# Attention and two gated layers on one core: score products by half tiles, one half ahead, and inverses handled by pairs of tiles

## What is computed

```
scores = scale * q @ k.T + bias          # bias: -slope[head] * distance, masked to -1e9
a = exp(scores - max); a = a / (sum(a) + 1e-9)
x = (a @ v), heads joined                          # [2, 768, 512]
gate = sigmoid(causal conv over 5 positions of x)
x = (gate * (x @ w_val)) @ w_out
h = relu(x @ w_in)
gate = sigmoid(conv over 3 positions of h)
out = (h * gate) @ w_out2
```

## Time and profile before

| | us |
|---|---|
| median of 3 runs | 261.65 (261.6 to 261.84) |
| the profiled execution, device time | 260.86 |
| its span, first to last instruction | 259.1 |
| first turned tile on PE | 35.92 |
| `pv(10)` starts on PE | 87.02 |
| `val_part(0, 0)` starts on PE | 89.14 |
| PE busy in the whole span | 248.1 (96%) |

### The profile page before, as it was taken

The page is one execution under the profiler, slowest core; times in us unless marked ns, Lnnn a source line. Parts: engine busy times, 40 slices in busy tenths (PEclk is TensorE's granted clock), DMA queues, the critical chain, the costliest instruction groups (busy, mean ns, idle before and its releaser), DMA issues.

```text
span 259.1 us, 4771 instructions
## 1 busy us (share of the span) xinstructions
PE 248.1 (96%) x1702; PEld 199.7 (77%) x1702; DVE 183.4 (71%) x469; ACT 147.8 (57%) x346; POOL 46.8 (18%) x71
## 2 busy tenths in 40 slices
PE   8999989989789899999999999999999999999995
PEld 7644558888688778888888888888888888888883
DVE  0388369998989988989805969986139989990000
ACT  1061649999999854455517058855458559662100
POOL 1002255777478612000000000000000000000000
PEclk9999999999999999999999999999999999999999
DMA  6799957897976120000000000000000004004021
GB/s 204 266 341 270 287 199 202 248 239 229 271 220 202 57 74 4 0 4 0 0 0 3 0 0 0 1 3 0 0 0 3 0 0 162 3 0 162 0 115 47
DMA packets 24636, 24.69 MB, mean 95 GB/s; under 512 B 3732, under 2 KB 16532, under 8 KB 24484
## 3 DMA queue, kind: packets, MB, share of 16 engines
q1 hardware_dynamic: 23460, 23.37, 29.8%
q10 hardware_dynamic: 1152, 1.01, 1.2%
HBM read 21.03 MB, written 3.34 MB: 94 GB/s over the span
## 4 chain that ended last, share of the span: by engine, by line
PE 84%; ACT 9%; DVE 5%; issue 2%
PE ps L592 21%; PE ps L594 21%; PE ps L593 21%; PE ps L478 9%; ACT prob L732 6%; PE ps L559 3%; DVE prob L982 3%; PE ps L525 2%; PE ps L563 2%; ACT probT L739 2%; PE ps L493 2%; PE ps L489 1%; DVE probT L989 1%; DVE xT L1005 1%; ACT Wh L720 0%
## 5 line engine op out<-in xcount | busy, mean ns | idle before, releaser
L732 ACT ACTIVATE prob<-prob,low 128x232 f32<-128x232 f32 (+1 forms) x96 | 44.2, 465 | 4.9 <-DVE low L982 4.8
L1010 DVE SCALAR_TENSOR_TENSOR g<-xT,cw,g 128x512 f32<-128x512 f32 x48 | 34.7, 787 | 1.6 <-ACT g L767 1.6
L838 ACT ACTIVATE h<-ps 128x512 f32<-128x512 f32 x24 | 14.0, 596 | 31.2 <-PE ps L594 31.1
L982 DVE CUSTOM_DVE_ANT_0 prob<-ps,bias 128x232 f32<-128x232 f32 x80 | 28.0, 388 | 1.5 <-PE ps L525 1.5
L559 PE MATMUL ps<-probT,v_new 128*64 128x128 f32 x192 | 19.3, 280 | 6.5 <-ACT probT L739 6.5
L592 PE MATMUL ps<-gh,Wh 128*128 128x512 f32 x64 | 24.9, 389 | 0.0
L593 PE MATMUL ps<-gl,Wh 128*128 128x512 f32 x64 | 24.9, 389 | 0.0
L594 PE MATMUL ps<-gh,Wl 128*128 128x512 f32 x64 | 24.9, 389 | 0.0
L592 PE MATMUL ps<-hghA,w2h 128*128 128x512 f32 x64 | 24.9, 389 | 0.0
L593 PE MATMUL ps<-hglA,w2h 128*128 128x512 f32 x64 | 24.9, 389 | 0.0
L594 PE MATMUL ps<-hghA,w2l 128*128 128x512 f32 x64 | 24.9, 389 | 0.0
(11 more groups left out here) (110 smaller groups left out, 590.1 us busy)
## 6 DMA issues: line engine op xcount, KB each, us to landing
q_rows<-in_q SPq DMA_DIRECT2D x12, 256.0 KB, 4.3
kW<-in_k SPq DMA_DIRECT2D x12, 256.0 KB, 5.4
v_new<-in_v SPq DMA_DIRECT2D x12, 240.0 KB
invT<-inv_turned SPq DMA_DIRECT2D x20, 128.0 KB, 3.4
out<-xT SPq DMA_DIRECT2D x5, 512.0 KB, 2.8
w<-in_w SPq DMA_DIRECT2D x8, 256.0 KB, 9.3
v_old<-in_v SPq DMA_DIRECT2D x10, 192.0 KB
prob<-in_wval SPq DMA_DIRECT2D x1, 1024.0 KB, 4.9
```

The source lines that it names most:

```text
L732: act.activation(part, part, ACT.Exp, scale=-1.0, bias=low[:, t % 2, i:i + 1], accum_out=total[:, t % 2, i, 0:1]).then_inc(exp_done, 1)
L838: act.activation(h_cols(m, c), pieces(HB(m), c), ACT.Relu).then_inc(relu_done, 1)
L982: dve.tensor_tensor_reduce(prob[:, t % 2, i, cols], SC(f, e)[:, i % HH // 2, cols], table, -SCALE, 3.0e38, ALU.add, ALU.min, low[:, t % 2, ...
L1010: dve.scalar_tensor_tensor(out=pieces(g[:, m, :], c), in0=x_cols(m, c, tap - PAD1), scalar=cw1[:, m, tap:tap + 1], in1=pieces(g[:, m, :], ...
```

## The change

Scores are made by half tiles. PE no longer starts an iteration with the scores of tile t+1. It turns tile t, makes the first half of the scores of tile t+2, does `pv(t)`, and then makes the second half of tile t+2. DVE reads the four heads of the first half of tile t+2 at the end of iteration t, ahead of `take_x(t)`, so its iterations begin with the copies of the turned tile. The inverses of two tiles are made, stored and spread together, in odd iterations on DVE and SP; POOL scales two tiles in even iterations, starting at 2. `total` has four slots in place of two. ACT's order is not changed.

```diff
             def send_inverses(u):
+                slot = u % 2
+                sp.wait_ge(inverse_done, u + 1)
+                sp.dma_start(inv_turned[u].rearrange("h (b q) -> b h q", q=SQUARE), inv_rows[:, slot, :]).then_inc(inv_sent[slot], 16)
+
+            def spread_inverses(u):
+                slot = u % 2
+                sp.wait_ge(inv_sent[slot], 16 * (u // 2 + 1))
+                if u >= 1:
+                    sp.wait_ge(x_ready, 2 * u)
                 for e in range(2):
-                    sp.dma_start(invT_of(t)[e * D:(e + 1) * D, :, :], inv_turned[t, e:H:2, :].partition_broadcast(D)).then_inc(invT_in[slot], 16)
+                    sp.dma_start(invT_of_two(u)[e * D:(e + 1) * D, :, :], inv_turned[u, e:2 * H:2, :].partition_broadcast(D)).then_inc(invT_in[slot], 16)
...
                 for t in range(TILES):
-                    send_inverse(t)
+                    if t % 2 == 1:
+                        send_inverses(t // 2)
                     if t >= 1 and t - 1 + RING < TILES:
                         load_v(t - 1 + RING)
                     if t + RING < TILES:
                         load_q(t + RING)
                         load_k(t + RING)
-                    spread_inverse(t)
+                    if t % 2 == 1:
+                        spread_inverses(t // 2)
...
-                    if t >= 1:
+                    if t >= 2 and t % 2 == 0:
+                        scale_x(t - 2)
                         scale_x(t - 1)
+                scale_x(TILES - 2)
                 scale_x(TILES - 1)
...
                 for t in range(TILES - 1):
-                    if t >= 1:
-                        qk(t + 1)
                     for f in range(HALVES):
                         turn(t, f)
+                    if t + 2 < TILES:
+                        qk_half(t + 2, 0)
                     pv(t)
+                    if t + 2 < TILES:
+                        qk_half(t + 2, 1)
...
+                for i in range(HH):
+                    score(1, i)
                 for t in range(TILES - 1):
-                    if t >= 1:
-                        take_x(t - 1)
-                    score(t + 1, 0)
-                    score(t + 1, 1)
-                    inverse(t)
-                    score(t + 1, 2)
-                    turn_inverse(t)
                     copy_t1(t, 1)
-                    score(t + 1, 3)
+                    if t % 2 == 1:
+                        inverses(t // 2)
                     copy_t1(t, 3)
+                    if t % 2 == 1:
+                        turn_inverses(t // 2)
                     for i in range(HH, H):
                         score(t + 1, i)
+                    if t + 2 < TILES:
+                        for i in range(HH):
+                            score(t + 2, i)
+                    take_x(t)
                     for _ in range(EARLY_STEPS.get(t, 0)):
                         early_conv1(next_step)
                         next_step += 1
-                take_x(TILES - 2)
-                inverse(TILES - 1)
-                turn_inverse(TILES - 1)
+                inverses(TILES // 2 - 1)
+                turn_inverses(TILES // 2 - 1)
```

More of the change, by code:

```diff
@@ L125, in program @@
         low = sb("low", [P, 2, H], where=am)
-        total = sb("total", [P, 2, H, 2], where=am)
-        total_eps = sb("total_eps", [P, H], where=am)
+        total = sb("total", [P, 4, H, 2], where=am)
+        total_eps = sb("total_eps", [P, 2, H], where=am)
         inv = sb("inv", [P, SQUARE], where=am)
@@ L135, in program @@
         attention_memory.close()
[L136 removed]
+        inv_turned = nc.dram_tensor("inv_turned", (TILES // 2, SQUARE, P), f32, kind="Internal").ap()
         gm = ExitStack()
@@ L511, in _, with qk_half @@
             product_W(CT + 1)
+            def qk_half(t, f):
+                slot = t % RING
+                if f == 0:
+                    pe.wait_ge(q_in[slot], landed(t))
+                    pe.wait_ge(k_in[slot], landed(t))
+                    pe.wait_ge(k_window, k_windows(t))
+                if t >= 1:
+                    pe.wait_ge(score_done, H * (t - 1) + HH * (f + 1))
+                for i in range(HH):
+                    pair, rows = 2 * f + i // 2, slice(i % 2 * D, i % 2 * D + D)
+                    keys = kW[rows, slot, pair, OLD if first_of_batch(t) else 0:KEYS]
+                    last = pe.matmul(SC(f, i % 2)[:, i // 2, OLD if first_of_batch(t) else 0:KEYS], q_rows[rows, slot, pair, :], keys,
+                                     start=True, stop=True)
+                last.then_inc(qk_done, 1)
             def qk(t):
-                slot = t % RING
-                pe.wait_ge(q_in[slot], landed(t))
-                pe.wait_ge(k_in[slot], landed(t))
-                pe.wait_ge(k_window, k_windows(t))
                 for f in range(HALVES):
-                    if t >= 1:
-                        pe.wait_ge(score_done, H * (t - 1) + HH * (f + 1))
-                    for i in range(HH):
-                        pair, rows = 2 * f + i // 2, slice(i % 2 * D, i % 2 * D + D)
-                        keys = kW[rows, slot, pair, OLD if first_of_batch(t) else 0:KEYS]
-                        last = pe.matmul(SC(f, i % 2)[:, i // 2, OLD if first_of_batch(t) else 0:KEYS], q_rows[rows, slot, pair, :], keys,
-                                         start=True, stop=True)
-                    last.then_inc(qk_done, 1)
+                    qk_half(t, f)
             def turn_bank(t, j):
```

41 lines of the change are left out of this document (17 added, 24 removed).

## The result

The changed kernel takes **264.94 us** (median of 4 runs, 263.04 to 267.02), the kernel before, on the same chip in the same minutes, 261.62 (4 runs, 260.95 to 261.84). The ratio is 1.0119, with a 95% interval of 1.0081 to 1.0157. So the change costs some 1%, where I had forecast a gain of 0.5%. A second measurement, made later with six runs, gave 262.87 against 260.77, a ratio of 1.0092 (1.0056 to 1.0127): again slower, by somewhat less. All ratios here leave out executions more than 1.5% above the fastest of their kernel (here the one of 267.02 us), so they are not quite the quotients of the medians.

What follows compares the result with a forecast made beforehand. ACT, nearly full, bounds the attention loop. 2.5 us won, less 0.2 (late DVE copies), 0.3 (convolution beside POOL) and 0.8 (key windows), gives 1.2: 261.65 - 1.2 = 260.4 us, range 259.2 to 262.0.

Steps and rivals of the forecast that it cites:

- What bounds the loop, and what can be won: Attention loop: ACT nearly full, 4.67 us of work in rounds of 5.03; at most 2.5 us to win.
- Window 6: POOL's key window for tile 6: done at 56.8, wanted at 54.8, PE stands 2.0, 0.8 us lost.
- Later ones are in time by 0 to 1 us: POOL's key windows after 7 and 8, which are late without further cost: in time by 0 to 1 us.
- landing of 4.4 us: Key load 5, from issue at 44.10 to its window's start at 48.54; reused for the changed kernel.
- Storing and spreading: Inverses of two tiles: issue 0.62 per spread taken, 1.24 as bound, landing as before; cost 0.
- The cover of 0.15: Tile 6: pair 1 scaled by 63.8, ACT asks for x_ready 4 at 63.95, leaving 0.15 us.
- rival B: ACT stands at x_ready 4 in iteration 5: 261.15 in mildest form, 263.05 with a 2.6 us wait; chance 0.15.
- DVE and the convolution steps: Late iterations: late DVE copies cost pv(10) 0.2 us; convolution steps beside POOL cost 0.3, ends 0 and 1.2.
- forecast 5.3: DVE's round in iteration 9, with a convolution step and the inverses: 5.3 us.
- The slack of 0.5: DVE before iterations 8 and 9: about 0.5 us built up, set against the longer rounds there.
- Rival D: Both convolution steps on DVE held off by POOL: 1.2 in place of 0.3, time 261.3; chance 0.10.
- Rival C: Circle through take_x binds: turn and hand-overs 1.2 not 0.75, round 5.0, 261.65 less 0 to 0.4; chance 0.10.

Runs made afterwards that it cites:

- second profile: Later profile of the unaltered changed kernel, span 261.0 at clock 1.000; its six runs gave 262.87 us, ratio 1.0092 to the kernel before.
- half_keys_first: Changed kernel with inverses tile by tile and SP's loads behind the store in order keys, queries, values: 260.44 us, ratio 0.9985 to the kernel before.
- pairs_keys_ahead: Changed kernel with key and query loads ahead of the inverses' store in SP's queue, values behind it: 260.04 us, ratio 0.9953 to the kernel before.
- pairs_few_values: Changed kernel with value transfers cut to 16 rows from tile 4 on: 261.74 us, ratio 1.0025 to the kernel before.
- half_only: Changed kernel's new score order on PE and DVE, but inverses tile by tile: 263.29 us, ratio 1.0076 to the kernel before.
- pairs_loads_first: Changed kernel with all loads of an iteration ahead of the inverses' store in SP's queue: 264.99 us, ratio 1.0147 to the kernel before.
- pairs_filler: Changed kernel with four unread matrix products on PE ahead of the scores of tiles 6 and 10: 266.06 us, ratio 1.0178 to the kernel before.
- pairs_windows_ahead: Changed kernel with keys and queries ahead of the store, and POOL's next key window ahead of the two scalings: 262.44 us, ratio 1.0054.

## Point by point: what the prediction had right and wrong

**What bounds the loop, and what can be won: right.** ACT ran without a wait from 35.84 to 55.67, in rounds of 4.65 (forecast 4.67), which won 1.09 us by tile 4 (forecast 1.02, the three gaps up to there).

**Window 6: place and cause right, the size differs between the two profiles.** Forecast: scalings over at 56.6 (measured 54.10 + 2.50 = 56.6), window done at 56.8 (57.58), PE stands 2.0 (2.14), lost 0.8 (2.01). Of the gap of 1.2, 0.8 is the window: it had to wait 0.77 for its keys, which I had put down as present. The rest is that my step swallowed 0.7 of the delay in tile 6's shorter exponentials; ACT stood 1.62 at the turn, not 0.5, and made up nothing. In the second profile the window is done at 56.69, PE stands 0.87 and 0.72 is lost: near the forecast, though with less of a wait.

**The failed step: "Later ones are in time by 0 to 1 us", and the landing of 4.4 us under it.** I had one landing time, of key load 5 in the kernel before, and used it for all key loads and, in effect, for the spread (56.6 to about 61). The trace before already had key loads of 3.1 to 6.0 us; the changed kernel has 3.5 to 8.0. And the step is about every window from 7 on, but no row was worked out for any of them. PE stood 2.04 us at window 10 in the first profile, 1.88 at window 9 and 1.60 at window 10 in the second. From long landings came the 0.77 at `x_ready`, the 0.87 at window 10 and 0.8 of window 6. Putting keys and queries earlier in SP's queue, with nothing else changed, takes the loss away (`half_keys_first`, `pairs_keys_ahead`), and fewer bytes take most of it: so keys that come too late for the new order are the cause. Why they land later with pairs is open. The 6.9 us in which SP is silent, which I first took for it, put off 0.2 MB, and `pairs_keys_ahead` lands as late without that backlog.

**Storing and spreading: the price of the issue right, the landing not.** Two issues took 1.28 to 1.34 us, about as the 1.24 of before, though each transfer is twice as large. Pair 1 was spread at 56.70 (forecast 56.6), but it landed near 63.0, 6.3 us later instead of about 4.4. The cover of 0.15 was far too thin for that; ACT stood 0.63 (0.82 in the second profile). This was rival B in its mildest form.

**DVE and the convolution steps: right in kind, together 0.9 in place of 0.5.** DVE in order of time, late iterations, against the earlier trace rows.

```profile
82.96 0.59 DVE L1002 COPY probT<-ps 128x416 f32<-128x416 f32 x1
...
87.63 1.22 DVE L1023 SCALAR_TENSOR_TENSOR g<-xT,cw,g 128x512 f32<-128x512 f32 x1
88.78 1.18 DVE L1002 COPY probT<-ps 128x416 f32<-128x416 f32 x2
```

From one copy to the next it takes 5.82 us in iteration 9, which is the forecast 5.3 plus 0.48 for a step that took 1.22 in place of 0.74. `pv(10)` starts behind DVE's copy, 1.00 idle. The slack of 0.5 that I had counted on had been used up at window 10. The long step ran while POOL had its cast from 87.69 on (0.61, as elsewhere) and then L436 from 88.39, which itself took 1.60 in place of 1.27. The Trainium skill (SBUF — State Buffer, section "SBUF: two separate sides") states an exclusive lock between a DVE operation with two SBUF inputs and a GpSimd operation that reads SBUF: whichever starts first holds it for the whole instruction. The trace agrees but for who came first: the step, whose row starts 0.06 before the cast's, took 0.48 longer, then L436 took 0.33 longer beside the step. The other step, at 82.11, took 0.74, and POOL's key window, started after it, 0.90 in place of 0.50. In the second profile both steps took 0.74, while `pairs_few_values` and `pairs_keys_ahead` each have one of 1.85 and 1.79. Rival D, both steps held off for 1.2, did not come true.

**Rival C,** that the circle through `take_x` binds throughout, is refuted by the rounds of 4.65.

**No rival for the keys.** My list had nothing slower than 263.05 and gave slower 0.10. What was missing is the case that the windows after the sixth are late too, because the scores ask for every tile's keys almost an iteration earlier while SP's queue brings them no earlier.

## What to carry to other kernels

When an edit needs data earlier, work out for every tile when its load is issued, when it lands and when it is wanted, with the whole spread of landing times and not one of them: here 3.1 to 6.0 us before and 3.5 to 8.0 after, where I had used 4.4. Where a queue falls silent, add up the bytes from the start and not in the silent stretch alone: the view of 38 to 42 us showed 0.74 MB missing, the sum 0.2. And in such a queue order the loads by urgency around the store: the urgent ones ahead of it, enough others between it and the transfer that needs it, which here turned 1% slower into 0.5% faster (in one measurement).

## What the runs showed of the hardware that I had not expected

The time that one transfer of 256 KB needs to land is no constant of its size: the median of the key loads between 60 and 84 us was 3.9 us (`half_keys_first`, share of the main queue 78.4%), 4.4 (before, 77.8%), 5.4 (`half_only`, 90.6%) and 6.5 (after, 99.7%), at nearly the same GB/s (230 to 238); but it isn't set by that share alone, as `pairs_keys_ahead` had 7.1 at 92.3%. The way of a 16 KB store to memory, until the queue could go on, cost up to 4.5 us where nothing covered it (`pairs_loads_first`). And a fall of TensorE's granted clock from 1.00 to 0.50 came with stretches in which PE was busy for 0.91 (`pairs_filler`) or 1.78 of 4 us (`pairs_windows_ahead`), in some executions of a kernel and not in others, at about 2.2 us each in the latter kernel.
